# One slot for two pairs of heads beside the first product, in a fused attention and MLP kernel

## The reference

```python
scores = scale * np.matmul(q, k.transpose(0, 1, 3, 2))
scores = cap * np.tanh(scores / cap)
scores = scores - np.max(scores, axis=-1, keepdims=True)
attn = np.exp(scores)
attn = attn / (np.sum(attn, axis=-1, keepdims=True) + 1e-09)
out = np.matmul(attn, v)
...
h = x @ w_in
r = np.maximum(h, 0.0)
g = s * (r * r) + b
y = g @ w_out
```

## Time and profile before

| what | value |
| --- | --- |
| median of 3 runs | 592.5 us (592.3 to 593.12) |
| profiled execution | 592.38 us, its span 590.6 us |
| PE busy | 584.2 us, 99% |
| DVE busy | 429.5 us, 73% |
| ACT busy | 341.8 us, 58% |
| POOL busy | 185.1 us, 31% |
| DMA | 118.65 MB, mean 201 GB/s |
| granted PE clock | 1.0 throughout |

### The profile page before, as it was taken

The page is one execution under the profiler, slowest core; times in us unless marked ns, Lnnn a source line. Parts: engine busy times, 40 slices in busy tenths (PEclk is TensorE's granted clock), DMA queues, the critical chain, the costliest instruction groups (busy, mean ns, idle before and its releaser), DMA issues.

```text
span 590.6 us, 8838 instructions
## 1 busy us (share of the span) xinstructions
PE 584.2 (99%) x3080; PEld 469.3 (79%) x3080; DVE 429.5 (73%) x646; ACT 341.8 (58%) x407; POOL 185.1 (31%) x143
## 2 busy tenths in 40 slices
PE   8999999999999999999999999999999999999997
PEld 4335778668868777878777999999999999999997
DVE  5988899978678768769774133678878999775453
ACT  7986776775575676666752456546456445543330
POOL 0013976403434343434324332142333433000000
PEclk9999999999999999999999999999999999999999
DMA  8422445343555545454444978878667799854532
GB/s 286 166 94 94 120 148 166 123 132 150 191 199 188 198 165 220 169 206 178 179 174 155 322 261 294 300 267 285 230 245 261 246 344 322 288 173 125 172 111 92
DMA packets 61611, 118.65 MB, mean 201 GB/s; under 512 B 6464, under 2 KB 44160, under 8 KB 61568
## 3 DMA queue, kind: packets, MB, share of 16 engines
q1 hardware_dynamic: 61568, 118.09, 58.2%
HBM read 78.75 MB, written 39.32 MB: 200 GB/s over the span
## 4 chain that ended last, share of the span: by engine, by line
PE 95%; ACT 3%; DVE 1%; issue 1%; DVEq 0%; ACTq 0%
PE banks L758 14%; PE banks L760 13%; PE banks L759 13%; PE banks L797 12%; PE banks L798 12%; PE banks L796 12%; PE banks L703 9%; PE banks L659 6%; PE banks L725 2%; PE banks L683 1%; PE banks L605 1%; ACT e L957 1%; ACT e L907 1%; PE banks L816 1%; PE banks L736 0%
## 5 line engine op out<-in xcount | busy, mean ns | idle before, releaser
L758 PE MATMUL banks<-x_hi,w_hi 128*128 128x448 f32 x384 | 142.6, 371 | 0.0
L760 PE MATMUL banks<-x_hi,w_lo 128*128 128x448 f32 x384 | 140.4, 366 | 0.0
L759 PE MATMUL banks<-x_lo,w_hi 128*128 128x448 f32 x384 | 140.3, 365 | 0.0
L797 PE MATMUL banks<-x_lo,w_hi 128*128 128x448 f32 x336 | 122.7, 365 | 0.0
L796 PE MATMUL banks<-x_hi,w_hi 128*128 128x448 f32 x336 | 122.7, 365 | 0.0
L798 PE MATMUL banks<-x_hi,w_lo 128*128 128x448 f32 x336 | 122.7, 365 | 0.0
L758 PEld LDWEIGHTS banks<-x_hi,w_hi 128*128 128x128 f32 x384 | 72.1, 188 | 20.3 <-issue 14.0
L964 ACT ACTIVATE hidden_sb<-banks 128x448 f32<-128x448 f32 x56 | 30.6, 546 | 99.2 <-PE banks L760 99.1
L982 ACT ACTIVATE x_hi<-e,beside 128x448 fp32r<-128x448 f32 x64 | 48.8, 763 | 49.8 <-PE banks L798 49.8
L760 PEld LDWEIGHTS banks<-x_hi,w_lo 128*128 128x128 f32 x384 | 72.1, 188 | 6.0
L957 ACT ACTIVATE e<-e,beside 128x1792 f32<-128x1792 f32 (+1 forms) x48 | 76.1, 1606 | 1.2
(11 more groups left out here) (129 smaller groups left out, 802.5 us busy)
## 6 DMA issues: line engine op xcount, KB each, us to landing
t_scratch<-work SPq DMA_DIRECT2D x32, 448.0 KB, 3.2
e<-t_scratch SPq DMA_DIRECT2D x64, 224.0 KB, 3.8
hidden_scratch<-hidden_sb SPq DMA_DIRECT2D x56, 224.0 KB, 1.9
work<-hidden_scratch SPq DMA_DIRECT2D x24, 448.0 KB, 4.4
e<-hidden_scratch SPq DMA_DIRECT2D x48, 224.0 KB, 4.0
beside<-q_k SPq DMA_DIRECT2D x23, 448.0 KB, 4.7
work<-w_out SPq DMA_DIRECT2D x16, 384.0 KB, 3.6
s_scratch<-work SPq DMA_DIRECT2D x16, 384.0 KB, 2.9
```

What stands on the lines that cost most here:

```text
L758: nc.tensor.matmul(out, w_hi[:, j, w], x_hi[:, batch % 2, c, :], start=c == 0, stop=False)
L759: nc.tensor.matmul(out, w_hi[:, j, w], x_lo[:, batch % 2, c, :], start=False, stop=False)
L760: last = nc.tensor.matmul(out, w_lo[:, j, w], x_hi[:, batch % 2, c, :], start=False, stop=c == CT - 1)
L797: nc.tensor.matmul(out, w_tile(w_hi_flat, i, k, d), ring(x_lo, n), start=False, stop=False)
```

## The change

Two pairs share one slot. `tiles_beside` now takes a quad and gives its batch and tiles: in the first batch tiles 0 and 1 (EARLY) come before pair 7's scores, 2 to 4 (up to AHEAD = 5) behind them, then three slots with 4, 4 and 3 tiles; the later batches have 5, 5 and 6. In a slot TensorE runs: scores of p+2 (last third in banks 4 and 5), values of p and of p+1, the tails, tail scores of the next quad in banks 4 and 5, scores of p+3 (last third in banks 6 and 7), and then the tiles. In the last slot there are no scores; three tiles stand between the values of pair 22 and those of 23. SPLIT becomes 8, so pair 7, the eighth, has plain scores. The odd pair's x goes through the buffer turned in place of xt, so that two scales follow each other. The first two stores of hid stand ahead of the loads of w_in's pieces 10 to 13, and the later loads stand two by two behind single stores. The combinations run two to a slot, from the second quad of batch 1 on. The work is the same but for pair 7's scores.

```diff
-FIRST_ENDS = (4, 6, 9, 11, 13, 16)
-ENDS = (3, 5, 8, 11, 13, 16)
+AHEAD = 5
+FIRST_ENDS = (9, 13, 16)
+ENDS = (5, 10, 16)
+ALONE = 3
...
-SPLIT = PAIRS + 1
+SPLIT = PAIRS + 2
...
-COMBINE = PAIRS + 4
+COMBINE = QUADS + 1
...
+            load_qk(PAIRS + 3)
+            for j in range(EARLY):
+                store_hidden(j)
+            for piece in range(CT + 4, CT + 8):
+                load_w_in(piece)
+            load_v(PAIRS + 2)
+            load_qk(PAIRS + 4)
+            for j in range(EARLY, AHEAD):
+                store_hidden(j)
+                for piece in range(CT + 8 + 2 * (j - EARLY), CT + 10 + 2 * (j - EARLY)):
+                    load_w_in(piece)
...
+            def free_for_last(p):
+                if p % 2:
+                    pe.wait_ge(x_done, p - 1)
+                else:
+                    batch, tiles = tiles_beside(p // 2 - 1)
+                    pe.wait_ge(relu_done, batch * JT + tiles.start)
...
+                if p >= PAIRS:
+                    pe.wait_ge(last_read, last_group(p - p % 2 + 1))
...
+            scores_of(PAIRS + 1)
+            for j in range(EARLY, AHEAD):
+                for c in range(CT):
+                    hidden_chunk(0, CT * j + c)
+            for quad in range(QUADS, B * QUADS):
+                p = 2 * quad
+                follows = quad + 1 < B * QUADS
+                if follows:
+                    scores_of(p + 2)
+                batch, tiles = tiles_beside(quad)
+                values(p)
+                if not follows:
+                    for j in tiles[:ALONE]:
+                        for c in range(CT):
+                            hidden_chunk(batch, CT * j + c)
+                    tiles = tiles[ALONE:]
+                values(p + 1)
+                tail_values(p, 2)
+                if follows:
+                    pe.wait_ge(last_read, last_group(p + 2))
+                    tail_scores(quad + 1, G1)
+                    scores_of(p + 3)
+                for j in tiles:
+                    for c in range(CT):
+                        hidden_chunk(batch, CT * j + c)
...
-                if p == PAIRS:
-                    split_high(SPLIT)
                 last_tanh(p)
                 exponential(p, 1)
+            split_high(PAIRS + 2)
             for j in range(EARLY):
                 rectify(j)
...
+                if SPLIT <= p + 4 < ALL:
+                    split_high(p + 4)
+                if follows:
+                    first_tanh(p + 2)
+                    last_tanh(p + 2)
+                    tails_tanh(p + 2)
+                    exponential(p + 2, 0)
+                    exponential(p + 2, 1)
+                    first_tanh(p + 3)
+                    last_tanh(p + 3)
+                rectify(batch * JT + tiles[0])
+                if follows:
+                    exponential(p + 3, 0)
+                    exponential(p + 3, 1)
+                rectify(batch * JT + tiles[1])
+                if SPLIT <= p + 5 < ALL:
+                    split_high(p + 5)
+                for j in tiles[2:]:
+                    rectify(batch * JT + j)
...
+                if SPLIT <= p + 3 < ALL:
+                    split_low(p + 3)
+                scale_two(p)
+                if SPLIT <= p + 4 < ALL:
+                    split_low(p + 4)
+                if follows:
+                    sums_of(p + 2)
+                if follows:
+                    invert(p + 2)
+                if follows:
+                    sums_of(p + 3)
+                if follows:
+                    invert(p + 3)
```

More of the change, by code:

```diff
@@ L261, in tails_group, with tiles_beside, slot_of @@
             return (p - PAIRS) // 2
-        def tiles_beside(batch, c):
-            ends = FIRST_ENDS if batch == 0 else ENDS
-            first = EARLY if batch == 0 else 0
-            return range(ends[c - 1] if c else first, ends[c])
-        def first_tiles(batch):
-            return [tiles_beside(batch, c).start for c in range(PAIRS) if (batch + 1) * PAIRS + c + 1 < ALL] if batch < B - 1 else []
+        def tiles_beside(quad):
+            batch, c = divmod(quad, QUADS)
+            ends = FIRST_ENDS if batch == 1 else ENDS
+            first = AHEAD if batch == 1 else 0
+            return batch - 1, range(ends[c - 1] if c else first, ends[c])
+        def slot_of(batch, j):
+            for quad in range((batch + 1) * QUADS, min((batch + 2) * QUADS, B * QUADS - 1)):
+                if tiles_beside(quad)[1].start == j:
+                    return quad
+            return None
         def stays(n):
@@ L302, in w_in_of, with x_of @@
             return tensor[:, f * JPP:(f + 1) * JPP, c * P:(c + 1) * P]
+        def x_of(p):
+            return turned if p > PAIRS and p % 2 else xt
         def acc(step, d):
```

162 lines of the change are left out of this document (75 added, 87 removed).

## The result

The changed kernel took 595.66 us (median of 7 executions, 593.81 to 596.12); the kernel before, beside it on the same chip, 593.07 us (7 executions, 592.3 to 593.28). The ratio is 1.0041, 95% interval 1.0032 to 1.0050: slower by 2.6 us, twice what a measurement of this kernel can tell from no change. The profiled execution of the changed kernel took 595.73 us, its span 593.9, against 592.38 and 590.6 before.

The account below looks back on a forecast made before the run. TensorE's own instruction stream was taken as the bound. TensorE alone -1.3 us (joins -1.7, plain scores +0.4), w_in wait +1.2 and VectorE's waits +1.7 make +1.6 on 592.38: 594.0 us, own range 592.8 to 595.5, overall 590.8 to 597.0.

Parts of the forecast that it names:

- Joins: TensorE's changeovers between operations in the slots: fewer with two pairs per slot, -1.7 us, between -0.7 and -2.2.
- Rival D: TensorE's slots: the change does not save joins, the unseen ones costing what the removed did; 595.0 us, inside the forecast's range.
- Plain scores: Pair 7's scores on TensorE: plain fp32 takes 2.46 us for twelve passes instead of 2.05, +0.4 us.
- New wait 1: Tile 4 of hid, ahead of the slots: TensorE waits for GpSimd's split of w_in to piece 11, +1.2 us, 0 to 2.2.
- New wait 2: VectorE's round in the slots: TensorE's odd scores wait for qk_lo or the scales, +1.7 us in all, 0 to 4.
- third slot (+1.0 predicted): VectorE's round there takes 31.25 us from the slot's start against a deadline of 30.3: +1.0 us, 0 to 2.7.
- first slot (+0.3): VectorE has two inverts in a row there, so split_low(9) and the scales end near their deadlines: +0.3 us, 0 to 1.
- the second (+0.4): Second slot: VectorE's round beside w_in's split takes 26.2 us where 26.1 is allowed; +0.4 us, 0 to 1.5.
- Rival B: Only w_in waits; a later first slot gives VectorE time and the third round fits: 592.3 us, no change; chance 0.12.
- Rival C: VectorE and GpSimd block each other for whole operations, lengthening sums in the slots: 598.3 us, 596.5 with half; chance 0.15.
- Rival A: Joins are saved and nothing waits, neither on w_in nor on VectorE's third round: 591.1 us, faster; chance 0.20.
- Costed at nothing: Slots and last stage: tail scores' wait, rectify against tile 2, stores' cover on SP, last stage's sums; all priced at zero.

Follow-up runs that it names:

- the kernel without waits: Changed kernel with loads of w_in's pieces 10 to 13 before the first two stores and ScalarE casting pieces 6 to 9, pair 7 plain: 590.83 us, ratio 0.9970.
- all three: Changed kernel with w_in loads ahead of the first two stores, pieces 6 to 9 cast on ScalarE, and pair 7's scores split: 590.63 us, ratio 0.9966.
- loads first: Changed kernel with the loads of w_in's pieces 10 to 13 ahead of the first two stores of hid: 592.99 us, ratio 1.0003.
- two tiles ahead: Changed kernel with two tiles of hid ahead of the slots behind pair 7 instead of three (AHEAD 4): 593.63 us, ratio 1.0023.
- plain scores: Kernel before with only pair 7's scores made plain fp32, its cast and subtraction gone: 593.17 us, ratio 1.0005.
- stores first: Kernel before with only the first two stores of hid put ahead of the loads of w_in's pieces 10 to 13: 592.6 us, ratio 0.9996.
- one store first: Changed kernel with the loads of w_in's pieces 10 to 13 between the first and second store of hid: 593.22 us, ratio 1.0013.
- last pairs in one block: Changed kernel with w_in loads before stores and pieces 6 to 9 cast on ScalarE, plus the last two pairs' values unseparated (ALONE 0): 595.59 us, ratio 1.0040.
- two tiles ahead, casts, loads first: Changed kernel with w_in loads before stores, pieces 6 to 9 cast on ScalarE, and two tiles behind pair 7 (AHEAD 4): 593.49 us, ratio 1.0021.
- ScalarE's casts: Changed kernel with ScalarE casting w_in's pieces 6 to 9 in GpSimd's place, stores still ahead of loads: 594.89 us, ratio 1.0039.
- pair 7 split: Changed kernel with pair 7's scores on split operands again, its cast on ScalarE and subtraction on VectorE back: 596.59 us, ratio 1.0070.

## Why the prediction was right or wrong

The forecast was 594.0 us, slower at 0.48; it is 595.66, in the range of 590.8 to 597.0 but above the forecast's own 592.8 to 595.5. The sign was right; two of its terms were not, and they partly cancelled.

- **Joins, -1.7 predicted.** -2.23 us in the changed kernel, -2.58 in the kernel without waits, whose trace has one fewer of the delays of 0.4 us told of at the end. With all three edits it is -2.27. The mechanism is right and the size 0.5 to 0.9 short, beyond the -2.2 where its range ended: I priced each changeover and took values behind values as twice 2.40 us, where they take 4.66. Rival D (joins not saved) is out.
- **Plain scores, +0.4 predicted.** +0.41 in the trace, +0.45 in the experiment that makes this change alone, whose interval holds 0 as well.
- **New wait 1, +1.2 predicted, 0 to 2.2.** The place and the releaser were right, to 0.4 us in the time at which TensorE comes (71.08 against 70.66; the profiled execution starts the stretch 0.42 late). The size was not: 3.12 us. The step that failed is the end of the split, 71.85 predicted and 74.06 measured. The issue of piece 10 was right (63.55 against 63.78). Landing was put at 2.9 to 3.5 us, from loads that met no stores; behind two stores it took 3.9 to GpSimd's start. A store is not special in this: over all traces the load of piece 10 lands in 2.8 to 3.0 us where SP issued nothing within 3 us ahead of it, in 3.3 to 4.4 us right behind one or two stores, and in 3.4 to 3.9 us where it follows a load of qk by 1.1 us, with no store ahead. And the two pieces, 4.8 us of the earlier trace rows, took 6.4, since each now meets VectorE's sums and GpSimd's cast of 0.61 us becomes 1.56 and 1.29. Both errors have one root: I moved the split later in time and kept the durations it had where it was.
- **The clock, not in the prediction at all: +1.63 us.** A wait was priced at its own length. In 5 of the 7 executions the mean clock is 0.996 or 0.997; the two at 0.999 and 1.0 took 593.81 and 593.98 us, 1.8 us below the median of the others. So the median of the changed kernel is made of the wait, and a fall of the clock behind it.
- **New wait 2, +1.7 predicted, 0 to 4.** None in the changed kernel. Two things took it away. In the third slot (+1.0 predicted) the round is shorter than counted: from the start of the slot's first scores at 130.24 it ends at 28.3 us, not 31.25, with TensorE wanting it at 29.85. The scales' group takes 3.0 us instead of 4.3 and the first sums 142.03 to 145.46, 3.4 instead of 5.3, since the pair combination falls at 145.9 to 150.2, beside the inverse. In the first slot (+0.3) VectorE's two inverts in a row do not wait for TensorE, and wait 1 and the clock, 4.7 us, gave them time; but with the loads first it fits as well. In the second (+0.4) VectorE's round starts with TensorE's tails and gains no time by the delay; it is shorter, 24.3 us instead of 26.2, since less of it meets GpSimd's split of w_in. Rival B said "a later first slot gives VectorE the time it lacked": the outcome is B's, with a w_in wait of its own size, the reason only in part. The experiments show the wait standing behind: 0.8 us in the second slot with loads first, 2.5 to 2.8 us in the first with two tiles ahead. In the first slot itself it does not come (qk_lo(9) at 82.35 against 83.85 with loads first).
- **Rival C, 598.3.** The Trainium skill ("SBUF — State Buffer", Who interferes with whom) gives an exclusive lock between VectorE and GpSimd. Operations do stretch where the two meet, 1.09 to 2.07 us for a sum on VectorE (70.18 in the changed kernel's timeline) and 0.61 to 1.29 or more for a cast on GpSimd, as that rule has it. But VectorE's busy time fell from 429.5 to 405.1 us, with one subtraction of 1.1 us fewer, and GpSimd's from 185.1 to 165.6 with as many instructions: in the new order they meet less. The rule was right and would have served better on wait 1, where GpSimd pays, than on the third slot. Two figures of this part are off by their own terms: half of C's 6.0 us above 592.3 is 595.3, not 596.5, and the third slot with both sums beside GpSimd is 2.85 us late, not 2.7. Neither moves the forecast.
- **Rival A, 591.1, faster.** "The joins are saved and nothing waits" needed the loads ahead of the stores and four casts off GpSimd: 590.83 and 590.63 us. What it promised is what those kernels give.
- **Costed at nothing,** and rightly: the tail scores' wait, rectify against tile 2, the last stage (1354 records in both). The stores' cover on SP held here, but it is thin: where the last pairs stand in one block it is gone, with 1.3 us of wait.

## What to carry to other kernels

When a change moves work earlier, price every transfer and every operation that now feeds it in its new surroundings: behind which transfer the load stands in the queue, and beside which engine the operation runs. The durations of the old place are no guide in either direction: two pieces took 6.4 us instead of 4.8 on GpSimd, and VectorE's third round 28.3 instead of 31.25. Price a wait on TensorE by its length and, where it is as long as those here (2.5 us and more), by the matmuls behind it at the lower clock. And when a wait is removed, expect less than its length back where another engine is nearly late: undoing one of two late feeders gave 2.7 of 4.7 us where undoing both gave 4.8.

## What was not expected of the hardware

How long a wait lets the clock fall. Mean granted clock of the executions that the medians count, by the wait in the kernel's profiled one:

| kernel | TensorE's longest wait from pair 7's scores on, us | executions with clock 0.997 or less |
|---|---|---|
| before; plain scores; stores first; all three; casts and loads first | none | 0 |
| one store first | 0.9 | 0 of 9 |
| loads first | 1.0 | 0 of 11 |
| last pairs in one block | 1.3 | 0 of 8 |
| two tiles ahead | 2.5 | 4 of 11 |
| two tiles ahead, casts, loads first | 2.8 | 2 of 11 |
| changed kernel | 3.0 | 5 of 7 |
| ScalarE's casts | 3.0 | 5 of 6 |
| pair 7 split | 3.4 | 6 of 7 |

With waits of 1.3 us or less the clock stayed up in all, with 2.5 to 2.8 us it fell in 6 of 22 executions and with 3.0 us or more in 16 of 20, the same program one way or the other. Between 1.3 and 2.5 us there is one case, in the trace of the execution of 604.91 us: behind a wait of 1.79 us, to 334.13, which followed one of 0.90 us, to 328.43, the clock fell. The waits were measured in one execution of each kernel, so the link of wait and fall in the others is argued, not shown. The Trainium skill ("TensorE: Matmul & The Clock Gate", The HAM clock gate) says that an idle array falls to 1.2 GHz, and that the moment of a change varies between runs, since the monitoring runs freely and does not restart with the kernel. The rows at 0.50 agree with the level, the table with the varying moment; so do two traces: in the changed kernel the first matmul behind the wait is slow already (74.20), with two tiles ahead the distances widen only 0.9 us behind it (82.10, 82.99).

Values of two pairs in a row take 4.66 us, 0.14 less than twice one pair: a changeover is paid where the operation changes, not per pair. And a run of hid's matmuls is now and then 0.2 to 0.4 us longer than its count, with matmuls at 0.207 us instead of 0.203, in all kernels; in the execution of 604.91 us it is so from 338 us to the end, 5.1 us in all. Its cause is open.
